# A bias column of 16 floats cut to one in an attention and expert-layer kernel

## The reference

```python
# attention: 2 batches, 8 heads, 768 positions, head size 64
keep = (pos_k < 4) | ((0 <= pos_q - pos_k) & (pos_q - pos_k < 128))
a = softmax(where(keep, q @ k.T / 8, -1e9)); attn = a @ v
x = attn as [1536 tokens, 512]
# first layer: 4 experts, all tokens, weighted by normalised probabilities p
out = sum over e of p[:, e] * (relu(x @ w1[e]) @ w2[e])     # 512 -> 1024 -> 512
# second layer
h = out @ w_in; g = h * cos(h); result = g @ w_out          # 512 -> 2048 -> 512
```

## Time and profile before

| | us |
|---|---|
| median of 3 runs | 898.9 (896.22 to 901.43) |
| profiled execution | 898.9 |
| its span, first to last instruction | 897.1 |
| TensorE busy | 865.7 (97% of the span) |
| VectorE busy | 490.2 (55%) |
| ScalarE busy | 472.9 (53%) |
| GpSimd busy | 533.3 (59%) |

### The profile page before, as it was taken

How to read it: one execution, slowest core, us unless ns; L and a number is a source line. 1 busy time by engine, 2 the same in 40 slices (tenths; PEclk the granted TensorE clock), 3 DMA queues, 4 the chain that set the end, 5 groups by cost and what they waited for, 6 DMA issues and landing times.

```text
span 897.1 us, 14124 instructions
## 1 busy us (share of the span) xinstructions
PE 865.7 (97%) x4750; PEld 758.1 (85%) x4750; DVE 490.2 (55%) x1123; ACT 472.9 (53%) x1030; POOL 533.3 (59%) x409
## 2 busy tenths in 40 slices
PE   7997889999999999999999999999999999899998
PEld 5665568989988998998899899889889989888997
DVE  4978873333433333663344334335767567857656
ACT  5766745234333433633342343344678669768764
POOL 2565646656475577567546465794944766864550
PEclk9969979999999999999999999999999999999999
DMA  8345211211221121122112112212202211420201
GB/s 189 88 91 107 49 60 47 94 47 47 95 82 59 49 94 47 47 95 89 47 53 94 48 48 94 56 55 80 94 6 90 95 47 48 150 72 37 95 0 71
DMA packets 66437, 64.12 MB, mean 71 GB/s; under 512 B 40128, under 2 KB 40128, under 8 KB 66368
## 3 DMA queue, kind: packets, MB, share of 16 engines
q1 hardware_dynamic: 66368, 63.22, 23.0%
HBM read 59.81 MB, written 3.15 MB: 70 GB/s over the span
## 4 chain that ended last, share of the span: by engine, by line
PE 87%; DVE 8%; issue 2%; ACT 2%; DMA 0%; SPq 0%; ACTq 0%
PE scores L1200 10%; PE scores L1204 10%; PE scores L1202 10%; PE scores L1230 9%; PE scores L1232 9%; PE scores L1228 9%; PE bank L1230 5%; PE bank L1232 5%; PE bank L1228 5%; PE bank L1200 3%; PE bank L1204 3%; PE bank L1202 3%; DVE weights L851 3%; PE scores L1115 2%; PE bank L1146 2%
## 5 line engine op out<-in xcount | busy, mean ns | idle before, releaser
L462 POOL TENSOR_TENSOR w_lo<-w_raw,w_hi 128x512 fp32r<-128x512 f32 x96 | 128.5, 1348 | 184.9 <-ACT w_hi L588 184.9
L1200 PE MATMUL scores<-x_hi,w_hi 128*128 128x384 f32 x528 | 177.9, 337 | 5.3 <-ACT kept L620 3.9
L1204 PE MATMUL scores<-x_hi,w_lo 128*128 128x384 f32 x528 | 176.7, 335 | 0.0
L1202 PE MATMUL scores<-x_lo,w_hi 128*128 128x384 f32 x528 | 176.6, 334 | 0.0
L469 POOL TENSOR_TENSOR w_lo<-w_raw,w_hi 128x1024 fp32r<-128x1024 f32 x48 | 116.8, 2442 | 72.5 <-ACT w_hi L598 72.5
L598 ACT ACTIVATE w_hi<-w_raw 128x1024 fp32r<-128x1024 f32 x48 | 50.7, 1059 | 190.4 <-PE scores L1232 190.4
L1232 PE MATMUL scores<-w_hi,h_lo 128*128 128x512 f32 x384 | 149.7, 390 | 0.0
L1230 PE MATMUL scores<-w_lo,h_hi 128*128 128x512 f32 x384 | 149.7, 390 | 0.0
L1228 PE MATMUL scores<-w_hi,h_hi 128*128 128x512 f32 x384 | 149.4, 389 | 0.0
L1200 PEld LDWEIGHTS scores<-x_hi,w_hi 128*128 128x128 f32 x528 | 99.1, 188 | 8.2 <-issue 7.7
L979 DVE SCALAR_TENSOR_TENSOR acc<-scores,probs,acc 128x512 f32<-128x512 f32 x56 | 41.8, 749 | 116.3 <-PE scores L1232 116.3
(11 more groups left out here) (126 smaller groups left out, 1657.7 us busy)
## 6 DMA issues: line engine op xcount, KB each, us to landing
w_raw<-in_moe_w_dram SPq DMA_DIRECT2D x32, 1024.0 KB, 5.1
w_raw<-in_moe_w_in_dram SPq DMA_DIRECT2D x8, 1024.0 KB, 5.0
w_raw<-in_moe_w_out_dram SPq DMA_DIRECT2D x8, 1024.0 KB, 5.1
v_nat<-in_v_dram SPq DMA_DIRECT2D x12, 256.0 KB, 3.2
out_dram<-acc SPq DMA_DIRECT2D x12, 256.0 KB, 4.1
k_nat<-in_k_dram SPq DMA_DIRECT2D x11, 256.0 KB, 4.0
q_nat<-in_q_dram SPq DMA_DIRECT2D x11, 256.0 KB, 4.6
k_nat<-in_k_dram SPq DMA_DIRECT2D x2, 128.0 KB, 2.5
```

The lines of the kernel that those rows point to most:

```text
L462: nc.gpsimd.tensor_tensor(w1_slots(w1_lo, h % 2, part), w1_part(h % 2, part), w1_slots(w1_hi, h % 2, part).bitcast(F32), ALU.subtract)\
L1200: nc.tensor.matmul(target[:, 0:HALF], w1_hi[:, i, slot, d], x_hi[:, n - 1, d], start=first and d == 0, stop=False, skip_group_check=True)
L1202: nc.tensor.matmul(target[:, 0:HALF], w1_hi[:, i, slot, d], x_lo[:, n - 1, d], start=False, stop=False, skip_group_check=True)
L1204: last = nc.tensor.matmul(target[:, 0:HALF], w1_lo[:, i, slot, d], x_hi[:, n - 1, d], start=False, stop=d == 1, skip_group_check=True)
```

## The change

`quarter` is declared with one column in place of 16, and the activation that reads it takes the whole tile in place of its first column. The fill at L412, `nc.gpsimd.memset(quarter[:], QUARTER)`, is not edited, but it covers what the tile now has. Tiles declared behind `quarter` are placed from its new end.

```diff
@@ -113,8 +113,7 @@
         w1_sum = sb("w1_sum", [P, 3, 2, FS // 2])
         w2_raw = sb("w2_raw", [P, 4, DM])
         ident = sb("ident", [P, P])
-
-        quarter = sb("quarter", [P, 16])
+        quarter = sb("quarter", [P, 1])
         probs_in = sb("probs_in", [P, T, E])
         probs = sb("probs", [P, T, E])
         probs_sum = sb("probs_sum", [P, T])
@@ -660,7 +659,7 @@
             def cosine(n):
 
                 act.wait_ge(folded, n + 1)
-                nc.scalar.activation(angles[:, n % 3], angles[:, n % 3], ACT.Sin, scale=-TWO_PI, bias=quarter[:, 0:1])\
+                nc.scalar.activation(angles[:, n % 3], angles[:, n % 3], ACT.Sin, scale=-TWO_PI, bias=quarter[:])\
                     .then_inc(cosine_ready, 1)
```

## The result

The changed kernel takes 906.75 us (median of 7 runs, 904.28 to 909.05) against 898.18 (median of 7, 895.26 to 903.14) for the kernel before. The ratio is 1.0092, with a 95% interval from 1.0062 to 1.0121: slower by about 0.9%, where no change was forecast; 906.75 lies above the forecast's range of 893.5 to 905.

What follows compares the result with a forecast made beforehand. TensorE's matmul stream was taken to bound the expert layers, a chain of short steps attention. Fill, reader and addresses were 0 each: 898.9 - 0.0 - 0.0 + 0 = 898.9, stated as 899.0 us; range 893.5 to 905.

Steps and rivals of the forecast that it cites:

- What bounds the kernel: Whole kernel: expert layers are a stream of TensorE matmuls, attention a chain of short steps; 87% of the chain is TensorE.
- The fill and the reader: `quarter`'s memset, 112 ns once, and the cosine's 64 bias reads: nobody waits for the fill, reads unchanged; 0.0 us each.
- The addresses: Tiles behind `quarter` move down 32 bytes, to starts 32 past a multiple of 64; taken as 0 us.
- the upper bound: Moved tiles: one more 64-byte piece per row on `kept` waits, last store and first queries; together 1.0 us at most.
- The witnesses: Attention's exponentials, masking and weight loads from `weights`: equal lengths at starts 0, 16, 32, 48 past 64, so no cost.
- the first rival: Attention, 1 to 137 us: VectorE, ScalarE and DMA steps on moved tiles slow by some 8 us, to 907; chance 0.11.
- The odd-start rival: Attention's moved tiles: a start that isn't a multiple of 64 costs some 8 us, giving 907; chance 0.11.
- Attention in other step: Attention's VectorE/GpSimd meetings and TensorE's half-clock stretches fall differently: 893 or 905 us; chance 0.12 faster, 0.08 slower.
- What would show it: Changed profile: exponentials, masking, `h_hi` loads (188 ns), second-layer matmuls (389) as before; expert stage within 1 us of its length.
- The rule that spoke for a gain of 0.2 us: First queries' DMA into `k_nat`: 256-byte rows go from 12 beats to 11, 2.73 us become 2.50, sum 898.7.

Runs made afterwards that it cites:

- the square of four kernels: Kernel before; with `h_hi`, `h_lo` alone 32 bytes further (1.0097); with `w2_hi` and all behind 32 further (1.0011); changed kernel with 32 bytes ahead of `w2_hi` (905.45 us).
- the sweep: Kernel before with `h_hi` and `h_lo` 0 to 480 bytes further, another distance in each of 24 steps; pitch 227.2 ns unmoved, otherwise up to 234.2 ns.

## Why the prediction was wrong

- **What bounds the kernel**: right. The expert layers are TensorE's stream, and the whole loss lies in it.
- **The fill and the reader**: right. 100 ns for 112, off every path; the one-column tile with the tiles put back is at 1.0005.
- **The addresses**: right that they are all that is left of the change, and right which tiles move. Of those that TensorE reads in the expert layers it missed `acc`, which is loaded as weights in 48 transposes; they kept their pitch of 109 ns with `acc` 32 bytes nearer to `ident`, so it costs nothing. Wrong in what they cost, in this step: "A load of `h_hi` takes 188 ns beside a matmul of 389, so 3 ns on it would be hidden." Against the pitch of 227 ns, which is the room that a load really has, one of 191 ns would still fit. What fails is the idea that a price can only show as a longer load. The loads did not become longer at all: 187 ns after. The matmuls start later, which no length of a load shows. The sentence just ahead of it had the cause in hand (`h_hi` and `h_lo` move, what streams through doesn't) and took it for a relief; the upper bound then charged nothing to TensorE. The cost was +6.1 ns for each of 1728, 10.5 us, where the term said 0.
- **The witnesses**: rows 5 and 6 hold as rows, and the changed kernel repeats them. They were asked the wrong question. They tell of single operations at four starts; what counts is the distance of two tiles that TensorE reads at the same time, and for the two products no row of before shows two such distances. The upper end of 1 us was built from one more piece of 64 bytes per row on every engine but the one that bounds the kernel. The run with a move of 64 bytes and the square of four kernels refute the very idea of a bad start. One reading was wrong besides: the first rival takes the normalisation off as cleared by rows 5, which don't show it; in rows 11 it runs from 274 to 1935 ns.
- **The odd-start rival** at 907 came out at the right number by luck: it charged 8 us to attention, which got 0.4 us shorter in the profile, and to VectorE, ScalarE and DMA, whose moves cost nothing (0.9994).
- **Attention in other step**: its sum of normalisations is 43.2 us against 42.0, and it ends within half a microsecond. Not the cause.
- **What would show it**: the text did name the outcome in which it is wrong, a group of moved tiles with a new length; matmuls of the second layer at 389 were on the list of what stays, and they are at 394 to 396 in the median.

The rule that spoke for a gain of 0.2 us (the Trainium skill, "DMA: Bandwidth & Descriptors", section "How a descriptor splits into AXI transactions") stays undecided: the first queries were on the chain for 2.65 us against 2.73, in one profile each.

What the cause is underneath is argued only. TensorE streams one tile while it reads the next weights; that the price depends on the distance of the two modulo 256 bytes, and not on either start, looks like two reads meeting in the same part of the memory. No run shows the reads themselves. The Trainium skill, "SBUF — State Buffer", section "Who interferes with whom", gives TensorE two independent read ports, one for the stream and one for weight loads, and says that it never waits on anyone. Of other engines the traces agree, as far as they go: with them idle the pitch is no better (226.6 and 234.1 ns, above). That its two reads are independent of each other, the sweep does not bear out: with nothing changed but their distance, the pitch goes from 227.2 to between 228.9 and 234.2 ns. Whether it is a conflict of banks, and why the width matters, was not shown.

None of the versions beats the kernel before. Two put all of its speed back into the changed kernel, the unused tile and `h_hi` and `h_lo` returned alone (1.0005, 0.9994), and moving both partners together loses none (1.0011).

## What to carry to other kernels

Where TensorE is the bound and tiles are laid one behind the other, a change of a tile's size moves all tiles declared behind it, and with them the distances between what is streamed and what is loaded as weights; keep such pairs a multiple of 256 bytes apart (shown for float32r matmuls of 512 columns with a load for each; at 384 columns many other distances are as good), and put small tiles behind the large ones or fill them up. Judge a matmul by the pitch from start to start against its columns at the clock, and never take a change for free because the weight load is as short as before. To clear a suspicion about addresses, move one tile of a pair, then both: a test of the start alone can't see it.

## What the runs showed of the hardware that was not expected

- For 128x512 float32r matmuls at the full clock, 227 ns from start to start at a distance of 0 modulo 256 bytes between the streamed and the loaded tile, 228.9 at 192, 230.0 at 24, 230.7 at 8 and 232.4 to 234.2 at all others tried; 4 bytes are enough. The loads' own length stays at 187 to 188 ns in the median.
- For 128x384, 173.3 ns at more than half of the distances, 175.9 at 128 and 180.0 at 28, where the first product, with other tiles, had 177.6 in the mean for 28.
- At good distances the steady pitch is 13.4 and 13.3 ns over the columns' own time (226.7 - 213.3 and 173.3 - 160.0). At 512 columns and most other distances it is 20.1 over (233.4).
